# Thresholded attention and two MLPs on one core: normalization on ScalarE instead of GpSimd, no filler matmuls, later weight splits

## The reference

```python
scores = scale * np.matmul(q, k.transpose(0, 1, 3, 2))
thresh = np.max(scores, axis=-1, keepdims=True) - tau
scores = np.where(scores >= thresh, scores, -1000000000.0)
attn = np.exp(scores - np.max(scores, axis=-1, keepdims=True))
attn = attn / (np.sum(attn, axis=-1, keepdims=True) + 1e-09)
x = np.matmul(attn, v)                      # then (tokens, heads * 64)
h = x @ w_in;  x = (h * (1 / (1 + np.exp(-1.702 * h)))) @ w_out
h = x @ w_in2; out = (h * np.tanh(np.where(h > 20, h, np.log1p(np.exp(h))))) @ w_out2
```

## Time and profile before

| | us |
|---|---|
| median of 3 executions | 1191.14 (1187.62 to 1191.17) |
| the profiled execution, its time | 1191.17 |
| its span, first to last instruction | 1189.4 |

### The profile page before, as it was taken

How to read it: one execution, slowest core, us unless ns; L and a number is a source line. 1 busy time by engine, 2 the same in 40 slices (tenths; PEclk the granted TensorE clock), 3 DMA queues, 4 the chain that set the end, 5 groups by cost and what they waited for, 6 DMA issues and landing times.

```text
span 1189.4 us, 19967 instructions
## 1 busy us (share of the span) xinstructions
PE 1116.8 (94%) x7652; PEld 1066.6 (90%) x7652; DVE 797.0 (67%) x1404; ACT 638.9 (54%) x880; POOL 447.2 (38%) x782
## 2 busy tenths in 40 slices
PE   6777998899998999999999999999999999999998
PEld 5777898899998999999989999999898989899897
DVE  5887888688888888888888733566344443443343
ACT  4665655465554655556556412367556445654553
POOL 6867777466666665667666300000000000000000
PEclk9997999999999999999999999999999999999999
DMA  7622124133223323233322011630000000001000
GB/s 249 201 78 85 49 59 113 48 82 103 55 63 103 87 83 84 58 96 92 80 81 73 16 39 37 211 117 27 1 28 27 27 27 27 27 6 48 1 27 27
DMA packets 95119, 81.52 MB, mean 69 GB/s; under 512 B 47664, under 2 KB 80432, under 8 KB 95024
## 3 DMA queue, kind: packets, MB, share of 16 engines
q1 hardware_dynamic: 95024, 80.24, 23.1%
HBM read 66.06 MB, written 14.16 MB: 67 GB/s over the span
## 4 chain that ended last, share of the span: by engine, by line
PE 78%; DVE 13%; issue 3%; ACT 3%; POOL 2%; DMA 0%; SPq 0%; DVEq 0%; ACTq 0%; POOLq 0%
PE ps_s L676 17%; PE ps_r L571 15%; PE ps_r L592 11%; PE ps_r L699 9%; PE ps_r L462 7%; PE ps_t L446 5%; PE ps_s L437 5%; PE ps_t L699 4%; PE ps_t L592 3%; DVE e_buf L502 2%; DVE neg_max L494 2%; DVE pt_lo L515 1%; DVE g_lo L621 1%; PE ps_t L571 1%; DVE q_st L396 1%
## 5 line engine op out<-in xcount | busy, mean ns | idle before, releaser
L743 DVE COPY hidden<-ps_s 128x768 f32<-128x768 f32 x48 | 45.8, 956 | 170.5 <-PE ps_s L676 170.5
L571 PE MATMUL ps_r<-x_hi,wi_lo 128*128 128x256 f32 x544 | 159.7, 294 | 0.1
L571 PE MATMUL ps_r<-x_lo,wi_hi 128*128 128x256 f32 x544 | 155.1, 285 | 0.0
L571 PE MATMUL ps_r<-x_hi,wi_hi 128*128 128x256 f32 x544 | 155.0, 285 | 0.0
L545 POOL TENSOR_SCALAR e_buf<-e_buf,inv_sum,even_share 128x576 f32<-128x576 f32 x144 | 121.9, 847 | 77.4 <-DVE inv_sum L510 77.3
L482 ACT CAST pt_hi<-ps_t 128x640 fp32r<-128x640 f32 x144 | 100.0, 694 | 91.6 <-PE ps_t L446 87.9
L515 DVE TENSOR_TENSOR pt_lo<-ps_t,pt_hi 128x640 fp32r<-128x640 f32 x144 | 118.1, 820 | 33.8 <-ACT pt_hi L482 32.2
L592 PE MATMUL ps_r<-g_hi,wo_lo 128*128 128x256 f32 x464 | 135.8, 293 | 3.6 <-DVE g_lo L621 3.5
L477 ACT ACTIVATE e_buf<-ps_s,neg_max 128x576 f32<-128x576 f32 x144 | 107.1, 744 | 58.7 <-DVE neg_max L494 58.3
L446 PE MATMUL ps_t<-ident,e_buf 128*128 128x128 f32 x720 | 106.2, 280 | 29.0 <-DVE pt_lo L515 23.4
L592 PE MATMUL ps_r<-g_hi,wo_hi 128*128 128x256 f32 x464 | 131.5, 284 | 0.0
(11 more groups left out here) (97 smaller groups left out, 3098.2 us busy)
## 6 DMA issues: line engine op xcount, KB each, us to landing
k_ll_raw<-in_k SPq DMA_DIRECT2D x64, 288.0 KB, 2.8
v_st_raw<-in_v SPq DMA_DIRECT2D x64, 160.0 KB, 2.9
wi_lo_raw<-in_moe_w_in SPq DMA_DIRECT2D x16, 512.0 KB, 5.1
wo_lo_raw<-in_moe_w_out SPq DMA_DIRECT2D x16, 512.0 KB, 5.9
q_raw<-in_q SPq DMA_DIRECT2D x32, 192.0 KB, 3.0
x_lo_raw<-x_scratch SPq DMA_DIRECT2D x9, 512.0 KB, 4.3
x_scratch<-y_acc SPq DMA_DIRECT2D x9, 512.0 KB, 3.5
x_lo_raw<-x_scratch SPq DMA_DIRECT2D x6, 768.0 KB, 4.7
```

Source lines behind the costliest of these rows:

```text
L571: mm = pe.matmul(bank[:, part * CH:(part + 1) * CH], wi[w][:, k, f * P:(f + 1) * P], x[:, k, :], start=t == 0, stop=t == 3 * KT - 1)
```

## The change

The kernel gets four edits.

1. From step FRONT on, the normalization moves from POOL (`pool_norm`) to ACT (`act_norm`, an Identity activation with scale and bias per row). POOL keeps it for the first 16 steps.
2. ACT's slot is reordered: the exponential comes last, the normalization of the step before just ahead of it, and both behind the casts of K, Q, V, weights and MLP input.
3. `pe_idle` is gone, and the lo part of V is made by POOL for all heads.
4. Four of the second MLP's weight chunks (places 8 to 11 of W2_ORDER) move from the last two "down" pieces to behind group 0, and the four behind them one group later on ACT. DVE now takes W2_BEHIND[g] in group g itself.

```diff
         def pe_turn(pe, n):
-            pe.wait_ge(s["normed"], n + 1)
+            if n < FRONT:
+                pe.wait_ge(s["normed_first"], n + 1)
+            else:
+                pe.wait_ge(s["normed"], n - FRONT + 1)
...
-        def pe_idle(pe, g):
-            if g >= 1:
-                pe.wait_ge(s["pv_sum"], g)
-            for _ in range(5):
-                pe.matmul(ring_bank(("pv", g + 1))[:, 0:P], ident[:, :], ident[:, :], start=True, stop=True)
...
+        def act_norm(act, n):
+            e = e_buf[n % 3][:, 0:S]
+            act.wait_ge(s["inverted"], n + 1)
+            act.wait_ge(s["share_ready"], n + 1)
+            act.activation(e, e, ACT.Identity, bias=even_share[:, n % 4:n % 4 + 1],
+                           scale=inv_sum[:, n % 4:n % 4 + 1]).then_inc(s["normed"], 1)
...
         W2_WITH = {downs_alone[n]: W2_ORDER[a:b] for n, (a, b) in
-                   enumerate(((0, 0), (0, 1), (1, 2), (2, 4), (4, 6), (6, 8), (8, 10), (10, 12)))}
-        W2_BEHIND = {0: W2_ORDER[12:14], 1: W2_ORDER[14:16]}
+                   enumerate(((0, 0), (0, 1), (1, 2), (2, 4), (4, 6), (6, 8)))}
+        W2_BEHIND = {0: W2_ORDER[8:12], 1: W2_ORDER[12:14], 2: W2_ORDER[14:16]}
...
@@ ACT, one slot @@
-                if n >= FRONT + 2 and n - 3 in GROUP_AT:
-                    act_pv(act, GROUP_AT[n - 3])
-                if not turn_first and 0 <= n - 2 < N:
-                    act_p_hi(act, n - 2)
-                if 0 <= n < N:
-                    act_exp(act, n)
...
+                if n >= FRONT + 2 and n - 3 in GROUP_AT:
+                    act_pv(act, GROUP_AT[n - 3])
                 for u in V_PREP.get(n, []):
                     act_v_hi(act, u)
                 if n in W_SLOT:
                     act_w_hi(act, 0, W_SLOT[n])
+                if not turn_first and 0 <= n - 2 < N:
+                    act_p_hi(act, n - 2)
                 if n in X_HI:
                     act_x_hi(act, X_HI[n])
+                if FRONT <= n - 1 < N:
+                    act_norm(act, n - 1)
+                if 0 <= n < N:
+                    act_exp(act, n)
...
@@ DVE, second MLP @@
-                for c in W2_BEHIND.get(g - 1, []):
+                for c in W2_BEHIND.get(g, []):
                     dve_w2_lo(dve, c)
...
@@ POOL, one slot @@
-                if 0 <= n - 1 < N:
+                if 0 <= n - 1 < FRONT:
                     pool_norm(pool, n - 1)
...
                 for u in V_PREP.get(n, []):
-                    if u >= H:
-                        pool_v_lo(pool, u)
+                    pool_v_lo(pool, u)
```

More of the change, by code:

```diff
@@ L225, in thresholded_attention_two_mlps @@
         names = ("tau_in x_in y_out x2_in zeroed ident_ready ready "
-                 "q_hi k_hi v_hi q_lo k_lo v_lo_first v_lo w_hi w_lo w_lo_too w2_lo "
-                 "qk_done maxed thr_ready flagged share_ready exped masked eps_ready inverted normed turned "
+                 "q_hi k_hi v_hi q_lo k_lo v_lo w_hi w_lo w_lo_too w2_lo "
+                 "qk_done maxed thr_ready flagged share_ready exped masked eps_ready inverted normed_first normed turned "
                  "p_hi p_lo pv_done pv_half pv_sum "
@@ L403, in act_v_hi @@
             act.copy(v[:, :, 0:D], v_raw[u % 2][:, :, D:P]).then_inc(s["v_hi"], 1)
-        def dve_v_lo(dve, u):
-            v = v_st[u % 2]
-            dve.wait_ge(s["v_hi"], u + 1)
-            dve.tensor_tensor(v[:, :, D:P], v_raw[u % 2][:, :, D:P], v[:, :, 0:D].bitcast(F32),
-                              ALU.subtract).then_inc(s["v_lo_first"], 1)
         def pool_v_lo(pool, u):
@@ L452, in pe_pv @@
             pe.wait_ge(s["p_lo"], last + 1)
-            if u < H:
-                pe.wait_ge(s["v_lo_first"], u + 1)
-            else:
-                pe.wait_ge(s["v_lo"], u - H + 1)
+            pe.wait_ge(s["v_lo"], u + 1)
             ring_release(pe, ("pv", g))
@@ L545, in pool_norm @@
             pool.tensor_scalar(e, e, inv_sum[:, n % 4:n % 4 + 1], even_share[:, n % 4:n % 4 + 1], ALU.mult,
-                               ALU.add).then_inc(s["normed"], 1)
+                               ALU.add).then_inc(s["normed_first"], 1)
         def slot_of(pair):
@@ L831, in _ @@
                         pe_pv(pe, GROUP_AT[n - 3])
-                    pe_idle(pe, max([g for m, g in GROUP_AT.items() if m <= n - 3], default=-1))
                     continue
@@ L947, in _ @@
                     dve_g_lo(dve, pair)
-                for u in V_PREP.get(n - 1, []):
-                    if u < H:
-                        dve_v_lo(dve, u)
                 if n - 1 in W_SLOT:
@@ L995, in _ @@
             pool.wait_ge(s["tau_in"], 16)
-            for n in range(-1, N + 1):
-                if 0 <= n - 1 < N:
+            for n in range(-1, N):
+                if 0 <= n - 1 < FRONT:
                     pool_norm(pool, n - 1)
-                if 0 <= n < N:
+                if n >= 0:
                     pool_row(pool, n)
```

## The result

| | before | after |
|---|---|---|
| median | 1191.16 us (1187.62 to 1191.37) | 1232.42 us (1231.0 to 1237.72) |
| profiled span | 1189.4 | 1231.2 |

The ratio is 1.0362, with a 95% interval of 1.0325 to 1.0398. The direction was forecast and the size was not: 1206 with a range to 1222.

The account below looks back on a forecast made before the run. PE was taken to bound the middle stage, DVE a close second. Front -4, thin stretch 0, middle stage +11 and second MLP +8.1 gave +15.1 on 1191.17, so 1206 us; own range 1199 to 1213, wider range 1194 to 1222.

Parts of the forecast that it names:

- Second MLP: Moved weight splits make PE wait 1.7 us before the third up group and 5 before the fifth; +8.1 us.
- Slots 41 and 77: Middle-stage slots without a piece: mask 2.3 us later, PE's wait about 5 us; +4.6 us for both.
- The middle stage: 110 to 680 us, attention interleaved with first MLP: ACT's new order costs +11 us, bounds -9 to +26.
- four thin K and Q slots: Middle-stage slots 30, 61, 92, 123, each followed by a P V: 0.5 us each, +2 us.
- bound of +26: Upper bound of the middle-stage term: 0.5 us at each of the 52 K and Q slots.
- The normalization on ACT: Each normalization moved from POOL to ACT was to take 0.70 us, within 0.66 to 0.74.
- The front: 8 to 84 us, filler gone and V's lo part on POOL: -4 us, bounds -15 to +15.
- B: Rival: ACT paces the middle stage, mask waits half a microsecond at every K and Q slot; 1221 us, chance 0.14.
- D: Rival: faster, POOL was the hidden hold-up and the normalization's move frees the middle stage by 18 us; 1177, chance 0.07.
- A: Rival: only the second MLP's stall shows, DVE's spare 15% hides ACT's order in the middle stage; 1195 us, chance 0.19.
- C: Rival: PE's lower clock without filler paces the front, which grows by 6 us; 1216 us, chance 0.07.
- The sentence on clock and filler from the Trainium skill: Throttled clock is the default and activity releases it; in the front it spoke against removing the filler.

Follow-up runs that it names:

- e6: The changed kernel with the second MLP's weight-chunk schedule of before; 1.0305 of the time before, 6.7 us less than the change.
- e9: The kernel before with K's cast moved between `pt_hi` and the exponential in every slot; 1.0005 of the time before.
- e18: The kernel before with K's cast alone at its new places: ahead of P V copy and `pt_hi` in P V slots, elsewhere ahead of the exponential; 1.0058.
- e5: The changed kernel with K's cast moved back behind the exponential; 1.0125 of the time before, 28 us less than the change.
- e16: The kernel before with ACT's new order, normalization still on POOL, but K's cast behind the exponential; 1.0070 of the time before.
- e2: The kernel before with ACT's new order, normalization still on POOL; 1.0213 of the time before.
- e3: The kernel before with both normalization on ACT and ACT's new order, nothing else of the change; 1.0315 of the time before.
- e1: The kernel before with the normalization on ACT just ahead of the exponential, other casts in the old order; 0.9974 of the time before.
- e7: The kernel before with only the filler matmuls removed; 0.9992 of the time before.
- e8: The kernel before with V's lo part on POOL for all heads, filler kept; 0.9959 of the time before.
- e17: The kernel before with the casts of K and Q at their new places, other casts at the old ones; 1.0175 of the time before.
- e15: The changed kernel with `pt_hi` first in every slot, all else as changed; 1.0434 of the time before.

## Why the prediction was right in direction and wrong in size

**Second MLP: right, and at its place.** With the 32.8 us that the kernel is late there, the waits were forecast at 803.8 + 32.8 = 836.6, 1.7 long, and at 842.0 + 32.8 = 874.8, 5 long. PE's timeline after:

```profile
836.61 0.41 PE L670 MATMUL ps_s<-x_hi,wi_lo 128*128 128x384 f32 x1 [1.65 <-DVE hidden L737]
...
874.68 0.69 PE L670 MATMUL ps_s<-x_hi,wi_lo 128*128 128x384 f32 x1 [4.77 <-DVE x_lo L726]
```

and the 8 us behind the second:

```profile
874.00:878.00 4.00, 3.32 (x10) 3.32 (x11) 0.63 (x1) 3.97 (x3) 0.00 (x0) 0.50 0.00 0
878.00:882.00 4.00, 4.00 (x17) 4.00 (x17) 0.09 (x1) 0.13 (x1) 0.00 (x0) 0.66 0.00 0
```

The clock took 3.3 x 0.50 + 4 x 0.34 = 3.0 us where I had 1.7. With 1.65 + 4.77 of waits that is 9.4 against 9.0 in the trace; 8.1 was forecast and e6 gives 6.7 to 8.4.

**Slots 41 and 77: right in the mechanism, wrong in the wait.** Slot 77 after, which answers the earlier trace rows:

```profile
376.61 0.71 PE L443 MATMUL ps_t<-ident,e_buf 128*128 128x128 f32 x5
...
379.90 0.86 ACT L471 ACTIVATE e_buf<-e_buf,even_share,inv_sum 128x576 f32<-128x576 f32 x1
...
381.43 0.82 DVE L496 SCALAR_TENSOR_TENSOR e_buf<-ps_s,thr,e_buf 128x576 f32<-128x576 f32 x1 [2.53 <-ACT e_buf L464]
...
385.88 1.30 PE L443 MATMUL ps_t<-ident,e_buf 128*128 128x128 f32 x5 [2.77 <-DVE pt_lo L509]
```

From the transposes to the mask pass 4.82 us instead of 2.37, 2.45 later (2.3 forecast). But the transposes that waited before, the second set behind, come 9.27 us behind instead of 7.48, 1.8 and not 2.3, and PE's wait is 2.77, not 5: PE itself came later to them, having waited for the normalization (0.42 us) and the mask (0.72) on the way, so the delays lie partly side by side. Slot 41 is alike: the mask 5.01 us behind instead of 2.37, the second transposes 9.47 instead of 7.48, a wait of 2.25.

**The middle stage: the step that failed.** The prediction put its term at +11; the trace has +35.1. The step that failed reads "Where PE's slot is full (with a piece it takes over 4 us) nothing is late", with 0.5 us for each of four thin K and Q slots. Three things were missing.
- I took K's cast as ready when ACT came to it, since in the middle stage of before it never had to wait. It never had to because of what stood in front: with `pt_hi` ahead of it in every slot the wait is 2.3 us in all (e9), with the cast ahead of `pt_hi` where there is a P V it is 30.0 (e18). Of the 2.3 us of delay I had summed only durations; with the load wait it reached 5 in slot 131, a full slot with a P V. K's cast back behind the exponential gave 28 of the 41 us of the whole loss (e5).
- I took small delays as covered one by one. Singly they are: K alone -0.4 us in this stage (e18), the rest without K 6.5 (e16); together they are 21.9 (e2), with the normalization 35.7 (e3).
- I priced the clock only behind the one wait in the second MLP. In the middle stage it made 7.2 us of the 35.1 (3.2 in e6), and PE's restarts behind the waits another 6.4. I had put a bound of +26 on the stage from half microseconds of idle time, and the idle time did stay within it (+21.5); both of these stood outside the sum.

**The normalization on ACT** took longer than the 0.70 taken:

```profile
L471 ACT ACTIVATE e_buf<-e_buf,even_share,inv_sum 128x576 f32<-128x576 f32 x114 | 98.9, 867 | 4.7 <-DVE inv_sum L504 4.4
```

0.87 us, outside the 0.66 to 0.74 forecast: neither the cast nor the exponential of the same shape was a bound for an activation that takes scale and bias from tiles. It is 0.17 us more in each slot. Its own price is not this, since e1 gains.

**The front:** -4 forecast, -2.6 measured to step 20, but that it came near is luck, not my reasons. I had given the filler most of it; alone it is worth nothing (e7), V's lo part 5.6 (e8), and the order takes 3.8 back (e2). The clock from 8 to 84 us was to fall below 0.8; it was 0.89 in the change, though 0.73 in e7.

**Rivals.** B, ACT as the pacer, was nearest: the mask does wait for the exponential, 48 times. D's claim that the normalization's move frees the kernel is in part true (e1, -3 us; its second half shows in `g_lo`, 0.80 us before and 0.68 in e1) and did not outweigh the order. A fell: DVE's spare 15% hides each of K's moves, but not all moves together. C fell with e7. The sentence on clock and filler from the Trainium skill held in direction (0.91 to 0.73 in e7), with no effect on the time.

**What stays open:** in which slots the moves use up each other's slack, and why PE in the profiled e17 ran so much at the lower clock when e18, with waits much like it, did not.

## What to carry to other kernels

In an in-order queue ask of each moved instruction not only how long it takes but when its data lands: an instruction that never waited may have been shielded by those in front of it. Price a wait of TensorE three times, as idle time, as the restart behind it and as the clock that may follow. PE's busy time over the same count of matmuls between two marks of the program shows the last two together; the granted clock tells them apart. Several moves that each cost nothing can share one slack: test them together before adding them up. And take a bundle apart before rejecting it, since two parts of this one made a kernel 0.8% faster.

## What the runs showed of the hardware beyond this

TensorE's busy time for the same 4233 matmuls ran from 526.6 us (e9, granted clock 0.99) to 551.4 us (e15, 0.96). Of these 24.8 us 15.7 are the clock (9.6 against 41.0 us of the work at the lower level) and 9.1 are restarts. The drops are not tied to long waits only. Two stretches of the changed kernel in a row, and a third for comparison (columns as in the earlier trace rows):

```profile
450.00:455.00 5.00, 2.54 (x17) 1.93 (x17) 4.90 (x11) 3.41 (x7) 1.54 (x6) 0.91 0.66 203
455.00:460.00 5.00, 5.00 (x22) 4.96 (x23) 3.03 (x8) 2.38 (x5) 3.89 (x7) 0.50 0.12 28
565.00:570.00 5.00, 5.00 (x37) 5.00 (x36) 2.72 (x7) 3.19 (x6) 2.33 (x5) 0.83 0.46 138
```

From 450 to 455 us PE was busy half the time, with no wait above 1.53 us, and then ran 5 us at 0.50, the lower level, with no gap in it: 22 matmul records where the third has 37.
